# The first half of a batch in a new order, with some scaling moved from VectorE to ScalarE

## The reference

```python
# 1: linear attention with decay, 8 heads of 48
for t in range(S):
    cur = einsum('bhd,bhe->bhde', u * k_t, v_t)
    y_t = einsum('bhd,bhde->bhe', r_t, state + cur)
    state = w_t[..., None] * state + einsum('bhd,bhe->bhde', k_t, v_t)
# 2: x = y as (4, 768, 384); causal softmax attention of 4 experts (width 64);
#    the two experts with the highest gate logit count for a token
w = exp(sel - max(sel)); w /= w.sum() + 1e-9
a = exp(scores - scores.max()); a /= a.sum() + 1e-9
out += mask * w * (a @ v @ wo[e])
# 3: a token-shift feed-forward layer
xk, xr = mu_k * x + (1 - mu_k) * x_prev, mu_r * x + (1 - mu_r) * x_prev
out = sigmoid(xr @ w_r) * (relu(xk @ w_k) ** 2 @ w_v)
```

## Time and profile before

| | |
|---|---|
| median of 3 runs | 688.29 us (688.19 to 689.12) |
| the profiled execution | 687.9 us, its span 686.2 us |
| TensorE enters `experts_sum(0)` | 71.07 us |
| TensorE busy over the span | 672.7 us (98%) |
| VectorE, ScalarE, GpSimd busy | 397.8, 322.3, 153.0 us |

### The profile page before, as it was taken

The page is one execution under the profiler, slowest core; times in us unless marked ns, Lnnn a source line. Parts: engine busy times, 40 slices in busy tenths (PEclk is TensorE's granted clock), DMA queues, the critical chain, the costliest instruction groups (busy, mean ns, idle before and its releaser), DMA issues.

```text
span 686.2 us, 12324 instructions
## 1 busy us (share of the span) xinstructions
PE 672.7 (98%) x4800; PEld 443.6 (65%) x4800; DVE 397.8 (58%) x787; ACT 322.3 (47%) x805; POOL 153.0 (22%) x200
## 2 busy tenths in 40 slices
PE   7998999999999999999999999999999999999998
PEld 7876656766657665676656666676665666566554
DVE  7899986292856577546574829647387213561200
ACT  2456656424662266722665237662276323563340
POOL 7663610161203520026010522005320000000000
PEclk9999999999999999999999999999999999999999
DMA  9998500005200170000800053000000000000000
GB/s 237 308 343 229 156 0 1 1 13 161 100 1 1 58 214 2 1 1 25 247 2 1 1 151 122 1 0 2 35 1 0 1 25 12 0 2 12 24 0 34
DMA packets 36921, 43.35 MB, mean 63 GB/s; under 512 B 2560, under 2 KB 27264, under 8 KB 36608
## 3 DMA queue, kind: packets, MB, share of 16 engines
q1 hardware_dynamic: 36864, 42.57, 21.1%
HBM read 37.84 MB, written 4.72 MB: 62 GB/s over the span
## 4 chain that ended last, share of the span: by engine, by line
PE 94%; DVE 3%; POOL 1%; issue 1%; ACT 1%; DVEq 0%; POOLq 0%
PE bank L964 82%; PE bank L968 6%; PE bank L1132 3%; PE bank L1128 3%; DVE idec L683 1%; DVE shared L730 1%; DVE att L753 0%; DVE nmax L717 0%; ACT shared L467 0%; POOL rk_sb L363 0%; ACT shared L476 0%; DVE dec L675 0%; ACT ktok L519 0%; POOL rk_sb L361 0%; POOL state L335 0%
## 5 line engine op out<-in xcount | busy, mean ns | idle before, releaser
L964 PE MATMUL bank<-wv_sb,k_sb 128*128 128x384 f32 x384 | 139.4, 497 | 0.0
L964 PE MATMUL bank<-xk_sb,wk_sb 128*128 128x384 f32 x384 | 136.5, 498 | 0.0
L964 PEld LDWEIGHTS bank<-xk_sb,wk_sb 128*128 128x128 f32 x384 | 68.9, 190 | 44.8 <-issue 5.5
L964 PEld LDWEIGHTS bank<-wv_sb,k_sb 128*128 128x128 f32 x384 | 67.5, 190 | 38.8 <-issue 3.7
L683 DVE RECIPROCAL idec<-dec 112x260 f32<-112x260 f32 x48 | 82.8, 1754 | 0.6
L467 ACT ACTIVATE shared<-bank,nmax 128x128 f32<-128x128 f32 (+5 forms) x96 | 59.9, 630 | 42.3 <-DVE nmax L717 42.3
L394 POOL TENSOR_TENSOR state<-state,carry 112x512 f32<-112x512 f32 x20 | 22.0, 1102 | 247.6 <-DVE state L772 131.1
L964 PE MATMUL bank<-xT_sb,wqk_sb 128*128 128x384 f32 (+1 forms) x240 | 64.1, 424 | 0.6 <-ACT xT_sb L525 0.6
L507 ACT ACTIVATE att<-ident,bonus 128x128 f32<-128x128 f32 x192 | 58.1, 390 | 10.2 <-DVE bonus L691 10.2
L704 DVE TENSOR_TENSOR out_sb<-bank,sg_sb 128x384 f32<-128x384 f32 x24 | 13.4, 557 | 85.2 <-PE bank L964 84.9
L717 DVE TENSOR_REDUCE nmax<-bank 128x1 f32<-128x128 f32 (+5 forms) x96 | 55.4, 618 | 10.0 <-PE bank L964 8.6
(11 more groups left out here) (93 smaller groups left out, 925.5 us busy)
## 6 DMA issues: line engine op xcount, KB each, us to landing
rk_sb<-in_rk SPq DMA_DIRECT2D x24, 384.0 KB, 7.0
v_sb<-in_v SPq DMA_DIRECT2D x24, 256.0 KB, 7.5
w_sb<-in_wT SPq DMA_DIRECT2D x24, 227.5 KB, 5.2
r_sb<-in_rT SPq DMA_DIRECT2D x24, 224.0 KB, 5.1
k_sb<-in_kT SPq DMA_DIRECT2D x24, 224.0 KB, 6.2
out<-out_sb SPq DMA_DIRECT2D x24, 192.0 KB, 1.9
wk_sb<-in_w_k SPq DMA_DIRECT2D x1, 1536.0 KB, 13.1
wv_sb<-in_w_v SPq DMA_DIRECT2D x1, 1536.0 KB, 18.0
```

The lines of the kernel that those rows point to most:

```text
L964: return nc.tensor.matmul(out, lhsT, rhs, start=start, stop=stop)
```

## The change

Five things change.

1. All five lists of the first half (loads, GpSimd, ScalarE, VectorE, TensorE) have a new order. The loads put the weights `wqk`, `wvg` earlier, and `v` of chunk 2 and `rk` of chunk 3 later.
2. In the first half ScalarE scales the probabilities of each second expert (`scale_second`), by a factor that VectorE computes; VectorE scales the first expert alone.
3. ScalarE takes the first state sum (`first_state`) in place of `state_update(0)`.
4. `decayed(n)` is split in the first half into `hats_by_decay(n)`, which doesn't need the inverses, and `hats_by_inverse(n, half)`.
5. The gate's normalization (a reciprocal and a multiplication in each half) goes away; its sum is multiplied into the softmax's before the reciprocal that is taken anyway. `bonuses` of chunks 6 and 7 move behind `keys(1, 0)`. The warm-up matmuls are 32 in place of 36, and the two later groups of 4 and 2 are gone.

From the second list on, lines that are only removed are left out of the order lists below; before, chunk 2's `v` stood behind `wvg`, and then came w, r and k of chunks 3 to 5 (with rk of 3 behind chunk 3's), v of 3 to 5, and rk of 4 and 5.

```diff
@@ loads, in order
             load_w(0)
+            load_w(1)
+            load_rk(0)
             sp.dma_start(u_sb[:, :], u).then_inc(L_U, 16)
-            load_rk(0)
-            load_w(1)
             load_r_k(0)
             load_r_k(1)
             load_rk(1)
             load_w(2)
             load_v(0)
-            load_r_k(2)
-            load_rk(2)
-            load_v(1)
             sp.dma_start(wqk_sb[:, :, :], wqk).then_inc(L_QK, 16)
             sp.dma_start(wvg_sb[:, :, :], wvg).then_inc(L_VG, 16)
+            load_rk(2)
+            load_w(3)
+            load_r_k(2)
+            load_v(1)
+            load_w(5)
+            load_v(5)
+            load_v(3)
+            load_w(4)
+            load_r_k(3)
+            load_r_k(5)
+            load_r_k(4)
             load_v(2)
...
+            load_rk(3)
+            load_v(4)
+            load_rk(4)
+            load_rk(5)
@@ GpSimd, new order from chunk 1 on
+            products(1)
+            hats_by_decay(1)
+            hats_by_inverse(1, 0)
+            carry_product(2)
+            hats_by_inverse(1, 1)
+            products(2)
+            carry_product(3)
+            carried(0)
+            hats_by_inverse(2, 0)
+            hats_by_decay(2)
+            hats_by_inverse(2, 1)
+            hats_by_decay(3)
+            hats_by_inverse(3, 0)
+            carry_product(4)
+            carried(1)
+            hats_by_inverse(3, 1)
+            products(3)
+            hats_by_inverse(4, 0)
+            products(4)
+            products(5)
+            carried(2)
+            hats_by_decay(4)
+            carry_product(5)
+            hats_by_inverse(4, 1)
...
@@ ScalarE, new
+            def scale_second(m):
+
+                w = width(0, m)
+                act.wait_ge(factor_ready, m + 1)
+                a.activation(prob[:, m % 2, w:2 * w], prob[:, m % 2, w:2 * w], ACT.Copy,
+                             scale=factor[:, m:m + 1]).then_inc(prob_scaled_a, 1)
@@ ScalarE, new order of the attention part
+            diagonal(4, 0)
             exponentials(0, 0)
             keys_by_token(3)
+            gate_exponentials(0)
+            x_chunk(3)
+            exponentials(0, 1)
             keys_by_token(4)
+            scale_second(0)
+            scale_second(1)
             transposed(0, 0)
+            exponentials(0, 2)
+            diagonal(4, 1)
+            scale_second(2)
             first_output(0)
+            exponentials(0, 3)
             transposed(0, 1)
+            diagonal(5)
+            exponentials(0, 4)
             first_output(1)
             transposed(0, 2)
+            scale_second(3)
+            scale_second(4)
             first_output(2)
             transposed(0, 3)
             exponentials(0, 5)
...
@@ VectorE, scale(h, m)
-                d.tensor_scalar(rinv[:, two], rsum[:, two], 1e-9, None, ALU.add).then_inc(rinv_step, 1)
+                d.scalar_tensor_tensor(rinv[:, two], rsum[:, two], 1e-9, bc(gsum[:, m // QM:m // QM + 1], [P, 2]),
+                                       ALU.add, ALU.mult).then_inc(rinv_step, 1)
...
-                for e in range(2):
+                if h == 0:
+                    d.tensor_tensor(factor[:, m:m + 1], rinv[:, 2 * m + 1:2 * m + 2],
+                                    gate[:, m // QM, 2 * (m % QM) + 1:2 * (m % QM) + 2], ALU.mult).then_inc(factor_ready, 1)
+                for e in range(1 if h == 0 else 2):
@@ VectorE, new order (all of it from scan(2) on)
+            scan(2)
+            bonuses(1)
+            dve.wait_ge(const_ready, 1)
             masks(0)
+            inverse(2, 0)
             inverse(2, 1)
+            scan(3)
+            bonuses(2)
             masks(1)
+            inverse(3, 0)
+            inverse(3, 1)
             state_update(1)
+            scan(4)
             masks(2)
             inverse(4, 0)
             inverse(4, 1)
+            scan(5)
             bonuses(3)
+            state_update(2)
+            inverse(5, 0)
             bonuses(4)
+            masks(3)
+            maxima(0, 0)
             gate_weights(0, 0)
+            maxima(0, 1)
             gate_weights(0, 1)
             scale(0, 0)
+            maxima(0, 2)
             scale(0, 1)
             state_update(3)
+            maxima(0, 3)
+            bonuses(5)
+            inverse(5, 1)
             scale(0, 2)
+            maxima(0, 4)
             masks(4)
             scale(0, 3)
+            maxima(0, 5)
             state_update(4)
             scale(0, 4)
+            scale(0, 5)
             masks(5)
@@ TensorE, new order
+            keep_warm(18)
+            keep_warm(14)
             linear_scores(0)
             keys_by_token(0)
             update(0)
-            keep_warm(4)
             x_chunk(0)
             linear_scores(1)
             keys_by_token(1)
             first_projections(0)
             x_chunk(1)
+            update(1)
             linear_scores(2)
+            keys_by_token(2)
             first_projections(1)
             x_chunk(2)
+            linear_scores(3)
+            update(2)
             first_projections(2)
+            keys_by_token(3)
             score_step(0, 0)
+            x_chunk(3)
+            score_step(0, 1)
             keys_by_token(4)
+            score_step(0, 2)
             transposes(0, 0)
             update(3)
+            score_step(0, 3)
+            transposes(0, 1)
             output(0, 0)
             update(4)
             score_step(0, 4)
+            transposes(0, 2)
+            linear_scores(4)
+            output(0, 1)
+            score_step(0, 5)
             output(0, 2)
             transposes(0, 3)
             linear_scores(5)
             output(0, 3)
+            transposes(0, 4)
             x_chunk(4)
             output(0, 4)
+            transposes(0, 5)
             x_chunk(5)
             output(0, 5)
```

More of the change, by code:

```diff
@@ L50 @@
 LAST = NHF - 1
-WARM_UP = 36
 SUM_BANK = (0, 1, 4)
@@ L162, in build @@
         rinv = sb("rinv", [P, TILES])
+        factor = sb("factor", [P, STEPS])
         oT_sb = sb("oT_sb", [P, QM, TOK])
@@ L371, in carry_product, with hats_by_decay, hats_by_inverse @@
                                     ALU.mult).then_inc(carry_ready, 1)
+            def hats_by_decay(n):
+                c = n % NC
+                lo, mid, hi = c * P, c * P + HALF, (c + 1) * P
+                pool.wait_ge(decay_done, n + 1)
+                pool.wait_ge(rkw_loaded[c], 32 * (n // NC + 1))
+                g.tensor_tensor(r_sb[:, :, mid:hi], r_sb[:, :, mid:hi], dec[:, n % 2, 1, :, 0:HALF], ALU.mult)
+                g.tensor_tensor(k_sb[:, :, lo:mid], k_sb[:, :, lo:mid], dec[:, n % 2, 0, :, 0:HALF][:, :, ::-1], ALU.mult)
+            def hats_by_inverse(n, half):
+                c = n % NC
+                lo, mid, hi = c * P, c * P + HALF, (c + 1) * P
+                pool.wait_ge(idecay_ready, 2 * n + half + 1)
+                pool.wait_ge(rkw_loaded[c], 32 * (n // NC + 1))
+                if half == 0:
+                    g.tensor_tensor(r_sb[:, :, lo:mid], r_sb[:, :, lo:mid], idec[:, n % 2, 0, :, 1:SEG][:, :, ::-1], ALU.mult)
+                else:
+                    g.tensor_tensor(k_sb[:, :, mid:hi], k_sb[:, :, mid:hi], idec[:, n % 2, 1, :, 1:SEG], ALU.mult).then_inc(hats_ready, 1)
             def decayed(n):
@@ L519, in keys_by_token, with first_state @@
                 a.copy(ktok[:, U % 2, :, :].rearrange("p a r -> p (a r)"), bank[:, 4, 0:PAIRS * R]).then_inc(ktok_ready, 1)
+            def first_state():
+                act.wait_ge(upd_psum, 1)
+                for e in range(2):
+                    new = bank[ROWS[e], 5, :].rearrange("p (a x) -> p a x", a=PAIRS)[:, :, e * HV:(e + 1) * HV]
+                    i = a.copy(state[ROWS[e], 1, :, e, :], new)
+                i.then_inc(state_sum, 1)
             def x_chunk(n):
@@ L587, in _ @@
             keys_by_token(1)
+            first_state()
             diagonal(2)
+            x_chunk(1)
             first_projections(0)
-            x_chunk(1)
             first_projections(1)
+            keys_by_token(2)
             x_chunk(2)
@@ L813, in gate_weights @@
                     dve.wait_ge(gate_step, G + 6)
[L814 to L819, removed]
+                    d.tensor_scalar(gsum[:, :], gsum[:, :], 1e-9, None, ALU.add).then_inc(gate_ready, 1)
+                    dve.wait_ge(gate_ready, h + 1)
             def keys(h, m):
@@ L933, in _ @@
                 keys(h + 1, 0)
+                if h == 0:
+                    bonuses(NC)
+                    bonuses(NC + 1)
                 if has(h + 2):
@@ L1239, in _ @@
             keys_by_token(1)
-            update(1)
             first_projections(0)
             x_chunk(1)
+            update(1)
             linear_scores(2)
+            keys_by_token(2)
             first_projections(1)
             x_chunk(2)
+            linear_scores(3)
+            update(2)
             first_projections(2)
-            keys_by_token(2)
+            keys_by_token(3)
```

(14 more changed lines are left out.)

103 lines of the change are left out of this document (33 added, 70 removed).

## The result

The changed kernel takes 695.75 us (median of 4 runs, 694.75 to 698.82), the kernel before beside it 688.24 us: ratio 1.0114, interval 1.0100 to 1.0128. It is slower by 7.5 us, past the forecast of 691.3 and out of the range that ended at 693.3. The profiled execution took 698.8 us, the slowest of the four, so its trace shows the loss in its largest form: 10.9 us over the 687.9 before. Its mean granted clock of TensorE was 0.983; the other three runs had 0.993, 0.990 and 0.992.

What follows compares the result with a forecast made beforehand. The prediction took TensorE to bound the kernel behind experts_sum(0), and a mesh of VectorE and TensorE before it. It added 3.0 us of first-half delay to 687.9, giving 690.9, or 691.3 as median; range 686.5 to 693.3.

Steps and rivals of the forecast that it cites:

- The direction and the queue waits: First half: new queue order makes TensorE wait, experts_sum(0) 3.0 us later; slower given 0.60 in all.
- scale_second waits for scale, which stands behind inverse(5, 1): Attention step 3: ScalarE starts exponentials 3 at 56.4, 3.6 us late, and TensorE sits idle for 3.6 us.
- the walk-through: Attention steps followed call by call from score_step(0, 0) at 42.5 to experts_sum(0) at 74.1, against 71.07: +3.0 us.
- the clock falls in the 3.6 us gap: Rival, TensorE before score 4: some 4 us of work at 7/11 pace costs 2 us, 693.3; chance 0.12.
- moved the mask: Start of first half: masks(0), now behind bonuses(1), ends at 18.0 (before 16.5); x_chunk(0) waits for it.
- 1.14 us as such a gap in mid-kernel: Old trace, TensorE: only short mid-kernel gaps, such as 1.14 us, at a granted clock of 1.00.
- The late load of `rk` 3: GpSimd's queue: rk 3 lands near 34.8, delaying products(3) and the state for x_chunk(3); cost 0.8 us, bounds 0 and 2.
- Start of the attention: TensorE: score_step(0, 0) starts at 42.5, 1.3 us later than before; bounds 41.4 and 44.
- VectorE sets the pace: Rival, first half: VectorE's shed work and fewer shared waits gain 3 to 5 us, 683 to 685.5; chance 0.20.
- Behind `experts_sum(0)`: Later halves: the gate's edit brings nothing under TensorE's full queue; moved bonuses and later loads cost 0, at most 1.

Runs made afterwards that it cites:

- e10: Changed kernel with filling matmuls (results unused) in five TensorE gaps: 6 before x_chunk(0), 4, 6, 14 before scores 2, 3, 4, 7 before output(0, 3); 692.08 us.
- e13: e12 with scale(0, 2) also moved ahead of bonuses(5) and inverse(5, 1) on VectorE; 689.28 us, ratio 1.0011 to the kernel before.
- e12: Changed kernel with 6 filling matmuls at the start and scale_second(1), (2), (4) moved behind exponentials(0, 2), (0, 3), (0, 5) on ScalarE; 692.37 us.
- e2: Changed kernel with 14 filling matmuls in the 3.8 us TensorE gap before score_step(0, 4) alone; 693.02 us, ratio 1.0070 to the kernel before.
- e5: Kernel before with the change's warm-up alone: 32 matmuls in place of 36, groups of 4 and 2 gone; 688.03 us, ratio 0.9992.
- e9: Kernel before, old order, with ScalarE scaling second experts, the gate normalization folded in and the change's last stretch; 690.61 us, ratio 1.0015.
- e7: Kernel before, old order, with the work edits alone: ScalarE scales each second expert, gate normalization folded in; 688.37 us, ratio 0.9993.
- the tail alone: Kernel before with the change's last stretch alone: transposes before x_chunk for steps 4 and 5, ScalarE and VectorE to match; 687.50 us, ratio 0.9982.
- e3: Changed kernel with 6 filling matmuls before x_chunk(0) and 14 before score_step(0, 4); 693.70 us, ratio 1.0086 to the kernel before.
- e14: e12 with filling matmuls before score 2 (4), transposes(0, 2) (8) and score 5 (3); 692.44 us, ratio 1.0057 to the kernel before.
- e4: Changed kernel with 6 filling matmuls at the start and scale(0, 2) moved ahead of bonuses(5) and inverse(5, 1) on VectorE; 692.52 us, ratio 1.0055.
- e15: e9 with 7 filling matmuls in the 1.8 us wait before transposes(0, 4); 688.42 us, ratio 0.9997 to the kernel before.

## Why the prediction was wrong

**The direction and the queue waits: right.** The step "scale_second waits for scale, which stands behind inverse(5, 1)" gave exponentials 3.6 us late and a TensorE gap of 3.6; measured 3.63 and 3.79. At full clock (e10) the sum of the walk-through came out at 74.89 for 74.1, and 692.1 us for 691.3. e13 shows the cause by undoing it: with the long gap and e12's wait of 1.95 us gone, 689.3.

**The step that failed is the price and the chance of the clock.** The forecast's sum has no term for it. The rival "the clock falls in the 3.6 us gap" was given 0.12 and 2 us, from 4 us of work at 7/11 of the pace. In the profiled run it fell behind just that gap, and stayed at 1.2 GHz for 16.9 us, not 4, while TensorE was busy for 16.79 of them; e2 puts that fall at 4.9 us. It had fallen before too, for 6.9 us from 18.8 on, behind a wait of 1.37 us at `x_chunk(0)`. That wait is new: VectorE's first mask ends at 18.25 instead of 16.5, and in the old order `x_chunk(0)` starts without a wait even when `keep_warm(4)` is gone (e5, at 17.04). The prediction moved the mask and dropped the group that would have covered the wait, and priced nothing there. All falls together cost 7.3 us in the profiled run and 3.7 in the median. The 2 us were near the size of one short fall (2.5 us between e9's two groups), not of what the new order brings.

The prediction also read the old trace too kindly. It named 1.14 us as such a gap in mid-kernel; the longest, which the earlier trace rows leaves out, is 1.40:

```profile
54.74 0.66 PE L968 MATMUL bank<-ident,shared 128*128 128x128 f32 x4 [1.40 <-DVE shared L730]
```

The clock was 1.00 there, and the forecast took that for a property of the kernel. It was one of that run: the kernel before loses its clock too in a few of its runs. The Trainium skill, TensorE: Matmul & The Clock Gate, What's actually happening, states the fall to 1.2 GHz after idling; the trace agrees with it at 60 us, behind 3.79 us, so that fall should have had the larger chance. The falls behind waits of 1.37 to 1.98 us, in some runs and not in others, are what these traces add.

**The late load of `rk` 3: no cost.** Put at 0.8 us. In e10 GpSimd starts `products(3)` at 34.09, not 34.8, and has the state ready at 42.7, not 43.8; `x_chunk(3)` follows `score_step(0, 0)` at once, at 42.97. The 0.8 us it did not cost went elsewhere on the way to score 2, which stood at 47.50 for the 47.6 of the walk-through.

**Start of the attention: right at full clock.** 42.33 in e10 for 42.5. In the changed kernel itself 45.45; the rest is the first fall of the clock, which stretched the work from `x_chunk(0)` to the first projections.

**The rival "VectorE sets the pace": wrong for this order.** In the changed kernel VectorE idles 2.44 us before the maxima of step 4, and its order makes the long gap, not its load. e7 shed the work in the old order and gained nothing measurable; with the tail (e9) it made a new wait, and the median is 690.6 where the tail alone has 687.5.

**Behind `experts_sum(0)`: right.** 614.94 us for 615.13; together the gate's edit and the moved bonuses cost and bring nothing that can be told.

Left open: which waits make the clock fall in a given run, and how long a fall lasts. The same kernel had it in some runs and not in others (e9); 1.37 us were enough once while 1.40 us in the kernel before, and 1.98 us in e2, were not; and a fall lasted from 3 to 4 us (e9, e13) to 16.9.

## What to carry to other kernels

Before a wait is put into an in-order queue, look at what stands behind the call that it waits for, in both queues: here a small scaling in front of the exponentials, and an inverse in front of the scale that it needs, cost TensorE 3.8 us. Price a gap on TensorE at more than its length: a forecast that makes new gaps of the size seen here (1.4 to 3.8 us) owes a second sum at half clock for what follows, with a real chance, even where the old trace shows such a gap without a fall. Matmuls into a free PSUM bank tell whether a loss is the wait or the clock, once every gap is filled (e10); with some gaps filled the fall can come at another (e3, e14). Take the clock of several runs, not of the profiled one alone.

## What was not expected of the hardware

The granted clock fell to 0.50 behind a wait of 1.37 us in the changed kernel and stayed there for 6.9 us; in e4 it fell behind waits of 1.68 and 1.55 us. Behind 3.79 us it stayed for 16.9 us, with TensorE busy for 16.79. A wait of 1.98 us at the same place brought a fall in e3 and none in e2. At 0.50 a 384-column score took 1.65 us for 0.92, a linear score 2.08 for 1.16, transposes of 4 blocks 1.06 to 1.12 for 0.66. Runs of one kernel spread with it: 694.8 to 698.8 for the changed kernel, 687.9 to 690.8 for e9, but 687.9 to 689.1 for e15. The kernel before, beside these runs, lay at 687.6 to 693.2. Removing ten matmuls of warm-up with no other edit (e5) was harmless: 0.9992.
